# Retention and two feed-forward stages: attention scores of a head pair over 64 array rows each

## The reference, cut to what matters

```python
state = gamma[None, :, None, None] * state + np.einsum('bhd,bhe->bhde', k[:, :, t], v[:, :, t])
y[:, :, t] = scale * np.einsum('bhd,bhde->bhe', q[:, :, t], state)
```

## Time and profile before

| what | value |
|---|---|
| median of 3 runs | 1046.72 us |
| the three runs | 1046.56, 1050.99, 1046.72 us |
| span of the profiled execution | 1048.8 us, 15480 instructions; no other time of its own is recorded |
| PE busy | 1023.9 us, 98% |
| PE weight loads | 900.6 us, 86% |
| DVE, ACT, POOL busy | 460.4 (44%), 431.9 (41%), 90.4 us (9%) |
| mean granted clock of TensorE | 0.995 of full |

### The profile page before, as it was taken

The page is one execution under the profiler, slowest core; times in us unless marked ns, Lnnn a source line. Parts: engine busy times, 40 slices in busy tenths (PEclk is TensorE's granted clock), DMA queues, the critical chain, the costliest instruction groups (busy, mean ns, idle before and its releaser), DMA issues.

```text
span 1048.8 us, 15480 instructions
## 1 busy us (share of the span) xinstructions
PE 1023.9 (98%) x5496; PEld 900.6 (86%) x5496; DVE 460.4 (44%) x874; ACT 431.9 (41%) x776; POOL 90.4 (9%) x101
## 2 busy tenths in 40 slices
PE   6799999999998999999999999999999999999998
PEld 4489999999998999999999888888888888888886
DVE  3847635356352463433324653253253254244243
ACT  3445333243231442413223464364364264265255
POOL 5321110111001011100000000000000000000000
PEclk9999999999999999999999999999999999999999
DMA  7664331532314234313134403013012012012000
GB/s 229 210 217 146 106 108 52 166 114 93 119 46 138 98 113 136 111 51 120 66 115 135 137 21 101 1 60 100 0 60 90 10 60 90 10 60 91 11 21 31
DMA packets 75656, 95.51 MB, mean 91 GB/s; under 512 B 7248, under 2 KB 59728, under 8 KB 75600
## 3 DMA queue, kind: packets, MB, share of 16 engines
q1 hardware_dynamic: 71856, 81.11, 24.1%
q0 software_dynamic: 3744, 13.63, 3.9%
HBM read 64.04 MB, written 30.67 MB: 90 GB/s over the span
## 4 chain that ended last, share of the span: by engine, by line
PE 93%; DVE 2%; DMA 1%; ACT 1%; issue 1%; SPq 0%; POOL 0%; DVEq 0%; ACTq 0%; POOLq 0%
PE psum L284 28%; PE psum L286 28%; PE psum L285 27%; PE psum L521 3%; PE psum L531 3%; PE psum L609 2%; PE psum L513 1%; DMA w_raw<-weights 1%; PE psum L548 1%; DMA v_buf<-v_rows 0%; PE psum L501 0%; DVE w_gv_lo L936 0%; ACT L802 0%; DMA chunk_decay_t<-chunk_decay 0%; DVE probs L897 0%
## 5 line engine op out<-in xcount | busy, mean ns | idle before, releaser
L284 PE MATMUL psum<-xn_hi,w_gv_hi 128*128 128x384 f32 x768 | 267.1, 348 | 1.0 <-issue 1.0
L286 PE MATMUL psum<-xn_hi,w_gv_lo 128*128 128x384 f32 x768 | 258.4, 336 | 2.6 <-issue 2.6
L285 PE MATMUL psum<-xn_lo,w_gv_hi 128*128 128x384 f32 x768 | 257.7, 336 | 0.0
L764 ACT ACTIVATE silu<-psum 128x384 f32<-128x384 f32 x96 | 47.2, 492 | 283.6 <-PE psum L286 283.6
L284 PEld LDWEIGHTS psum<-xn_hi,w_gv_hi 128*128 128x128 f32 x768 | 145.2, 189 | 4.3 <-issue 3.4
L286 PEld LDWEIGHTS psum<-xn_hi,w_gv_lo 128*128 128x128 f32 x768 | 144.9, 189 | 2.9 <-issue 2.9
L285 PEld LDWEIGHTS psum<-xn_lo,w_gv_hi 128*128 128x128 f32 x768 | 145.3, 189 | 0.9
L998 DVE TENSOR_TENSOR act_buf<-psum,silu 128x384 f32<-128x384 f32 x96 | 53.5, 557 | 199.9 <-PE psum L286 116.7
L284 PE MATMUL psum<-act_hi,w_out_hi 128*128 128x512 f32 x288 | 114.2, 397 | 0.0
L286 PE MATMUL psum<-act_hi,w_out_lo 128*128 128x512 f32 x288 | 112.3, 390 | 0.0
L285 PE MATMUL psum<-act_lo,w_out_hi 128*128 128x512 f32 x288 | 112.3, 390 | 0.0
(11 more groups left out here) (82 smaller groups left out, 1453.2 us busy)
## 6 DMA issues: line engine op xcount, KB each, us to landing
act_dram<-act_buf SPq DMA_DIRECT2D x96, 192.0 KB, 1.8
act_raw<-act_dram SPq DMA_DIRECT2D x72, 256.0 KB, 2.8
w_raw<-weights POOLq DMA_DIRECT2D x26, 512.0 KB, 4.9
kq_buf<-k_t SPq DMA_DIRECT2D x32, 192.0 KB, 2.8
kq_buf<-q_t SPq DMA_DIRECT2D x64, 96.0 KB, 2.9
k_buf<-k_rows SPq DMA_DIRECT2D x32, 192.0 KB, 2.9
v_buf<-v_rows SPq DMA_DIRECT2D x32, 192.0 KB, 3.1
out<-out_buf SPq DMA_DIRECT2D x24, 256.0 KB, 2.0
```

What stands on the lines that cost most here:

```text
L284: pe.matmul(dst, w_hi, m_hi, start=start, stop=False)
L285: pe.matmul(dst, w_hi, m_lo, start=False, stop=False)
L286: return pe.matmul(dst, w_lo, m_hi, start=False, stop=stop)
L764: act.activation(silu[:, f % 2, :], psum[:, GATE[f % 2], 0:TB], ACT.Silu).then_inc(silu_ready, 1)
```

## The change

The padded queries go. `kq_buf`, `kq_hi` and `kq_lo` hold 128 columns of keys and 128 of queries, the two heads one above the other. Each head's scores are a product over its own 64 rows: keys of 64 partitions x 128 columns stationary, queries of 64 partitions x 128 columns moving. The two heads write to two PSUM banks. In batches 1 to 3 these are six matmuls of 128 columns, head by head in turn, in place of three of 256; in batch 0 two in place of one. The second bank comes from the one that the sum of squares uses, so the next scores wait for ACT's root and the sum waits for the mask of the scores before it; the very first sum uses bank 2. Zeros, their semaphore and one DMA in five of each load go; `decay_q` is one instruction of 128 partitions.

```diff
-    kq_buf = sb(a, "kq_buf", [P, NP, HC, 3 * P])
-    kq_hi = sb(a, "kq_hi", [P, 3 * P], F32R)
-    kq_lo = sb(a, "kq_lo", [P, 3 * P], F32R)
+    kq_buf = sb(a, "kq_buf", [P, NP, HC, 2 * P])
+    kq_hi = sb(a, "kq_hi", [P, 2 * P], F32R)
+    kq_lo = sb(a, "kq_lo", [P, 2 * P], F32R)
...
-        GATE, VALUE, SUM = (0, 1), (2, 3), 7
-        SCORES, KV, Y = 4, 5, 6
-        SCORES_0 = (4, 0)
+        GATE, VALUE, SUM, SUM_BANK_0 = (0, 1), (2, 3), 7, 2
+        SCORES, KV, Y = (6, 7), 5, 4
+        SCORES_0 = (6, 7), (0, 1)
...  SP, load_run
-                if is_first(b) and r < NP:
-                    sp.wait_ge(q_zeros_set, q + 1)
-                q_src = row(q_t[:, :, tokens], p)
-                for h in range(2):
-                    rows = slice(h * HD, (h + 1) * HD)
-                    sp.dma_start(kq_buf[rows, q, :, (h + 1) * P:(h + 2) * P],
-                                 q_src[rows, :].rearrange("d (c t) -> d c t", c=HC)).then_inc(done, DMA)
+                sp.dma_start(kq_buf[:, q, :, P:2 * P],
+                             row(q_t[:, :, tokens], p).rearrange("d (c t) -> d c t", c=HC)).then_inc(done, DMA)
...  GpSimd
-            for q in range(NP):
-                pool.memset(kq_buf[:, q, :, P:3 * P], 0.0).then_inc(q_zeros_set, 1)
...
-                for h in range(2):
-                    at_least(pool, q_decayed, 2 * n + h)
-                    rows = slice(h * HD, (h + 1) * HD)
-                    pool.tensor_tensor(q_dec[rows, r % 2, :, :],
-                                       kq_buf[rows, q, :, (h + 1) * P:(h + 2) * P],
-                                       q_decay_t[rows, q:q + 1, :].to_broadcast([HD, HC, P]),
-                                       ALU.mult).then_inc(q_decayed, 1)
+                at_least(pool, q_decayed, 2 * n)
+                pool.tensor_tensor(q_dec[:, r % 2, :, :], kq_buf[:, q, :, P:2 * P],
+                                   q_decay_t[:, q:q + 1, :].to_broadcast([P, HC, P]),
+                                   ALU.mult).then_inc(q_decayed, 2)
...  TensorE, scores
-                dst = psum[:, scores_bank(b, ch), 0:2 * P]
-                k, qs = slice(0, P), slice(P, 3 * P)
+                banks, k, qs = scores_bank(b, ch), slice(0, P), slice(P, 2 * P)
                 if is_first(b):
-                    mm = pe.matmul(dst, kq_buf[:, q, i, k], kq_buf[:, q, i, qs], start=True, stop=True)
+                    for h in range(2):
+                        rows = slice(h * HD, (h + 1) * HD)
+                        mm = pe.matmul(psum[:, banks[h], 0:P], kq_buf[rows, q, i, k], kq_buf[rows, q, i, qs],
+                                       start=True, stop=True)
                 else:
                     pe.wait_ge(kq_lo_ready, (b - 1) * BC + ch + 1)
-                    mm = split_products(pe, dst, kq_hi[:, k], kq_lo[:, k], kq_hi[:, qs], kq_lo[:, qs], True, True)
+                    pe.wait_ge(rms_ready, sums)
+                    for step, (w, m) in enumerate(((kq_hi, kq_hi), (kq_hi, kq_lo), (kq_lo, kq_hi))):
+                        for h in range(2):
+                            rows = slice(h * HD, (h + 1) * HD)
+                            mm = pe.matmul(psum[:, banks[h], 0:P], w[rows, k], m[rows, qs],
+                                           start=step == 0, stop=step == 2)
...  TensorE, group, ahead of sum_squares
+                    if not last:
+                        step_at = STEP_AT_0 if is_first(b) else STEP_AT
+                        pe.wait_ge(probs_ready, (b + 1) * BC + 1 + max(ch for at, ch in step_at.items() if at <= SUM_GROUPS[u]))
                     sum_squares(t + 1)
```

More of the change, by code:

```diff
@@ L98, in retention_moe_kernel @@
     GROUPS = 4 * FC
+    SUM_GROUPS = (2 * SUM_AT + 1, 2 * FC + 2 * SUM_AT + 1)
     def steps_at(*ranges):
@@ L188, in retention_moe_kernel @@
         consts_set = sem("consts_set")
-        q_zeros_set = sem("q_zeros_set")
         run_loaded = [sem(f"run_loaded{i}") for i in range(NP)]
@@ L273, in step @@
                     if g in step_at and not last:
-                        attention_step(b + 1, step_at[g])
+                        attention_step(b + 1, step_at[g], 2 * b + 1 + (g > SUM_GROUPS[0]) + (g > SUM_GROUPS[1]))
                     group(b, g // (2 * FC), g // 2 % FC, g % 2, last)
@@ L301, in retention_moe_kernel @@
                     (rms_g_col[:], rms_g), (ln_g_col[:], ln_g))
-        RUN_DMAS = 5
+        RUN_DMAS = 4
         def run_of(ch):
@@ L357, in load_run, with attention_step @@
                     sp.dma_start(buf[:, q, :], row(src[:, :, tokens], p)).then_inc(done, DMA)
-            def attention_step(b, ch):
+            def attention_step(b, ch, sums=0):
                 if ch < 1 or (ch - 1) % HC < HC - 1:
@@ L491, in _, with scores @@
         def _(pe):
-            def scores(b, ch):
+            def scores(b, ch, sums):
                 r, q, i, _ = run_of(ch)
@@ L533, in outputs, with attention_step @@
                 mm.then_inc(y_done, 1)
-            def attention_step(b, ch):
+            def attention_step(b, ch, sums=0):
                 if 0 <= ch < BC:
-                    scores(b, ch)
+                    scores(b, ch, sums)
                 if ch > 0:
@@ L547, in sum_squares @@
                 at_least(pe, rms_ready, t)
-                pe.matmul(psum[:, SUM, 0:TB], ones[:], sq[:, 0, :], start=True, stop=True).then_inc(sum_done, 1)
+                bank = SUM_BANK_0 if isinstance(t, int) and t == 0 else SUM
+                pe.matmul(psum[:, bank, 0:TB], ones[:], sq[:, 0, :], start=True, stop=True).then_inc(sum_done, 1)
             def group(b, u, f, g, last):
@@ L733, in root @@
                 act.wait_ge(sum_done, t + 1)
-                act.activation(sq[:, 1, :], psum[:, SUM, 0:TB], ACT.Sqrt, bias=eps_col[:],
+                bank = SUM_BANK_0 if isinstance(t, int) and t == 0 else SUM
+                act.activation(sq[:, 1, :], psum[:, bank, 0:TB], ACT.Sqrt, bias=eps_col[:],
                                scale=1.0 / D).then_inc(rms_ready, 1)
@@ L896, in mask_scores @@
                 dve.wait_ge(scores_done, b * BC + ch + 1)
-                dve.tensor_tensor(probs[:, ch % 2, :], psum[:, scores_bank(b, ch), 0:2 * P], mask_t[:, run_of(ch)[1], :],
+                one, two = scores_bank(b, ch)
+                dve.tensor_tensor(probs[:, ch % 2, :].rearrange("p (h n) -> p h n", h=2),
+                                  psum[:, one:two + 1, 0:P],
+                                  mask_t[:, run_of(ch)[1], :].rearrange("p (h n) -> p h n", h=2),
                                   ALU.mult).then_inc(probs_ready, 1)
```

## The result

The changed kernel takes 1077.27 us (median of 4, 1076.42 to 1080.66); the kernel before, on the same chip, 1048.20 us (median of 4). The ratio is 1.0265, 95% interval 1.0227 to 1.0302: slower by some 28 us. The forecast was 1066 with a range of 1050 to 1095; the side and the range hold, the likeliest case's own range of 1059 to 1072 doesn't. The kernel of experiment 11 has two groups of executions 17 us apart, and its ratio is made from the lower group alone.

A forecast was written before the change was run, and what follows sets the result against it. PE was taken to bound the kernel: +21.3 us for steps of batches 1 to 3, +0.4 for batch 0, -2 lead-in, -0.4 and +0.2 for waits, +19.5 on 1046.7, giving 1066 us, range 1050 to 1095.

The forecast's parts named there:

- the likeliest case: Whole kernel: full switch cost for row halves, 1066 us, own range 1059 to 1072, chance 0.51.
- The bound: Whole kernel: PE sets the time in the steady part, where each microsecond added to PE goes on the end.
- The step of batches 1 to 3, +0.32: Scores and switches in a step: 0.68 us in place of 0.36; with +0.12 in nine steps, +21.3 us in all.
- pairs: Both heads' score products side by side in batches 1 to 3: first pair 0.06 us, second and third 0.11 each.
- exit 0.20: Switch from row-half scores back to a full-array product in batches 1 to 3: 0.20 us.
- the entry of 0.20: Switch from full array to row-half scores in batches 1 to 3: 0.09 emptying plus 0.11 weight load.
- Rivals 1 and 2: Split products of 128 columns at plain float32 pace, 1093 us (0.20); the heads' products not side by side, 1090 us (0.06).
- Rivals 3 and 4: Row-half switch costs only emptying the array, 1051 us (0.11); row halves need no switch, 1043 or 1040 us (0.12).
- The lead-in, -2 us: Before the groups: earlier loads and a shorter POOL queue save 2 us, bounds -4 and +0.5.
- some four scores that lie on the chain in this part, 0.19 each: Batch 0 scores in the lead-in: the added PE time set against the gains from earlier loads.
- The rest: Remaining effects: shorter waits for `kq_lo` -0.4 us, new wait of the sum for the mask +0.2 at most, others hidden.

The follow-up runs named there:

- experiment 11: Kernel before, head 0's output product ahead of the state update and head 1's behind it in the first twenty steps; ratio of the lower group 0.9984.
- Experiment 1: Changed kernel with row halves only in batches 1 to 3; batch 0, zeros, loads and query decay as in the kernel before; 1070.66 us, ratio 1.0179.
- experiment 4: Changed kernel with the two half-array output products moved ahead of the state update, one switch fewer; 1063.78 us, ratio 1.0132.
- experiment 9: Kernel before, each 256-column score product of batches 1 to 3 cut into two of 128 over all rows, one head after the other; 1068.17 us, ratio 1.0182.
- 2: Changed kernel with row halves only in batch 0; batches 1 to 3, zeros, loads and query decay as in the kernel before; 1056.22 us, ratio 1.0063.
- 6: Changed kernel with the three score products of head 0 first, then the three of head 1; 1079.32 us, ratio 1.0253.
- experiment 8: Changed kernel with two extra full-array products of ones behind each of the first twenty steps; 1085.1 us, ratio 1.0335.
- 12: Kernel before, each score product of batch 0 cut into two of 128 columns over the whole array; 1047.09 us, ratio 0.9969.
- experiment 5: Changed kernel with twelve plain full-array products of ones ahead of the first scores; 1073.4 us, ratio 1.0171.
- experiments 3: Kernel before, each 256-column score product of batches 1 to 3 cut into two of 128 over all rows, heads alternating; 1064.23 us, ratio 1.0131.
- experiment 7: Kernel before, output products of batches 1 to 3 over the whole array, using values padded with zeros; 1043.46 us, ratio 0.9911.

## Why the prediction was right, and where not

- **The bound.** Right: PE, busy for 229.92 of 230 us from 360 to 590 us in the changed kernel.
- **The step of batches 1 to 3, +0.32.** Right in its sum and in each term that a row shows: pairs at 0.10 to 0.11, exit 0.20, and 0.37 for L517 behind rows; the entry of 0.20 is what is left of 0.48. Experiment 1 has it alone at +19 us (15 to 22) for 21.3 forecast; experiment 4 shows that the 0.20 belongs to the switch; experiment 9 that a product of 128 columns with its load costs 0.10 to 0.11 without row halves too. The Trainium skill, TensorEngine Tiling (Array Packing), section Key Properties, says that a change of tiling mode drains the engine. The runs agree that such a change costs time, by the 0.42 that moves from one product to another in experiment 4. The gain of up to 2x in the table of the same page of the Trainium skill, section Theoretical Speedup, isn't to be had here: by the sum, 0.06 of the 0.68 is a pair's own streaming, and the rest is the pace of the pairs and the switches.
- **Rivals 1 and 2.** Out: 0.62 for six narrow products (experiment 9), two loads per line in the timeline. **Rivals 3 and 4.** Out, by the scores at 0.48 and the 0.42 behind them.
- **The lead-in, -2 us.** This is the step that failed: measured +7.8 in the profiled executions, and 1.1 more in the first groups, outside its own bounds of -4 and +0.5. It is more than chance: the groups start at 57.96 to 59.21 us in the three traces with row halves in batch 0 and the old order of the step (the changed kernel, 2 and 6), and at 47.90 to 53.55 in the eight without row halves there. The gains it counted were there in part: `v_buf` is issued at 3.24 and not 4.53, but the first product, which waits for it, starts at 6.96 instead of 7.62, for 6.3 forecast (DMA was at 0.89 between its issue and its landing). What failed is "some four scores that lie on the chain in this part, 0.19 each": it priced the added PE time at the full clock and let the other engines go on setting the pace. The runs show PE at its lower level up to 45.4 us, a full step at 2.81 us, and PE alone on the chain from 6.96 us to there. The trace of before held the warning, with pieces of 0.73 and 0.85 at 19 us. Experiment 2 ties this to the row halves in batch 0. Too little work for the array isn't the reason (experiment 8), nor are short products alone (12). Nor is a cold start reason enough: in experiment 5 the clock rose first and fell again, though one of its four executions must have kept it for most of the lead-in. In the kernel before, twice as many switches bring 17 us in six of ten executions (11), and with one switch fewer in the changed kernel the clock stays down too (4). What holds the clock down is thus not found: whether row halves do more than the switches they bring stays open, and so does the upper group of experiment 11.
- **The rest.** The new waits cost nothing measurable: in the list of PE's waits no root stands ahead of scores and no mask ahead of a sum. A mask ahead of scores stands there once in batch 0, for 0.3 us, where the kernel before has 0.7. The waits ahead of the split scores fell from 0.9 us to 0.6 (0.3 for `kq_lo` and 0.3 with no releaser seen), for 0.4 less in the forecast.

The profiled spans differ by 30.2 us for 19.5 forecast: one term of -2 was near +9, and the others held. By the ratio of the runs it is some 28. The wide range held it by luck, since its upper part came from rivals 1 and 2, and both were wrong.

## What to carry to other kernels

Cutting a product's 256 columns to 128 doesn't halve its time if each product has a weight load of its own: here 0.12 us became 0.10 to 0.11, with row halves and without, and every change between full array and halves cost another 0.15 to 0.20. Count the switches of a loop in the chain, by comparing the same product behind a full one and behind a tiled one; then ask whether zeros over the whole array are cheaper, as they were here in experiment 7. And where the trace of before shows both levels of TensorE's clock, price extra TensorE time there at both, and ask which engine sets the pace at the lower one.

## What the runs showed of the hardware

- The clock stayed at its lower level for 38 us in which PE was busy without a gap, and every product took near double (0.73 for 0.42). "Busy" alone didn't raise it; a plain product of 384 columns in two records stood right ahead of the rise at 45.4 us.
- The lead-in with its products unchanged ended anywhere from 47.9 to 53.6 us (experiments 3 and 1), with the clock's drops at different places: some 5 us of an execution's time are decided there.
- The same stream of steps ran with a mean granted clock of 0.981 to 0.984 in three executions and of 0.995 in a fourth, 10 us shorter (experiment 5).
- Two row halves are two streams: the order of their products in the program didn't change the time (0.48 and 0.49).
